# First loads of a one-core kernel: query loads alone on ScalarE's queue, key-value products in three parts, dummy products in TensorE's first waits

## What is computed

```
kv  = einsum('bhsd,bhse->bhde', k, v)             # 8 batches, 8 heads, 576 rows, 64 wide
out = einsum('bhsd,bhde->bhse', q, kv)
x   = out / sqrt(mean(out*out, -1) + 1e-6) * g_norm     # heads side by side: 4608 x 512
x   = relu(x @ w_in)**2 @ w_out                   # 512 -> 2048 -> 512
logits = x @ w_gate + modality_bias[modality_id]; e = argmax(logits)
out[token] = softmax(logits)[e] * (relu(x @ w1[e]) @ w2[e])   # 8 experts, 512 -> 1024 -> 512
```

## Time and profile before

| | us |
|---|---|
| median of 3 runs | 1384.91 (1383.55 to 1385.52) |
| time of the profiled execution | 1386.27 |
| its span in the trace | 1384.4 |
| TensorE busy in the span | 1356.5 (98%) |
| TensorE weight loads busy | 1114.6 (81%) |
| VectorE busy | 814.8 (59%) |
| ScalarE busy | 566.7 (41%) |
| GpSimd busy | 496.8 (36%) |
| mean granted TensorE clock | 0.994 of full |

### The profile page before, as it was taken

The page is one execution under the profiler, slowest core; times in us unless marked ns, Lnnn a source line. Parts: engine busy times, 40 slices in busy tenths (PEclk is TensorE's granted clock), DMA queues, the critical chain, the costliest instruction groups (busy, mean ns, idle before and its releaser), DMA issues. The chain is left out here.

```text
span 1384.4 us, 20776 instructions
## 1 busy us (share of the span) xinstructions
PE 1356.5 (98%) x6951; PEld 1114.6 (81%) x6951; DVE 814.8 (59%) x1765; ACT 566.7 (41%) x1129; POOL 496.8 (36%) x589
## 2 busy tenths in 40 slices
PE   5999999999999999999999999998999999999997
PEld 5887888888888888888887887876788888888876
DVE  3456574574564673664564655546666666666665
ACT  3443334334243333333333333334445545455543
POOL 2643232222132132232232134504555555555541
PEclk9999999999999999999999999999999999999999
DMA  8644646657566666567465464778996113851260
GB/s 231 185 107 151 198 116 199 189 128 201 183 126 190 186 142 199 174 133 215 158 145 161 148 143 160 199 263 199 321 345 243 47 49 115 303 206 48 81 253 21
DMA packets 183398, 237.45 MB, mean 172 GB/s; under 512 B 58734, under 2 KB 101646, under 8 KB 183314
## 3 DMA queue, kind: packets, MB, share of 16 engines
q1 hardware_dynamic: 169010, 214.85, 52.4%
q0 software_dynamic: 9472, 19.96, 4.5%
q10 hardware_dynamic: 4832, 1.57, 0.5%
HBM read 148.07 MB, written 89.30 MB: 171 GB/s over the span
## 5 line engine op out<-in xcount | busy, mean ns | idle before, releaser
L670 POOL TENSOR_TENSOR stage<-stage,stage_hi 128x512 f32<-128x512 f32 x128 | 170.5, 1332 | 547.8 <-ACT stage_hi L1150 547.6
L1499 DVE TENSOR_TENSOR g_sb<-g_sb 128x512 f32<-128x512 f32 x144 | 101.3, 703 | 322.7 <-ACT g_hi L1214 322.7
L1212 ACT ACTIVATE g_sb<-ps_h 128x512 f32<-128x512 f32 x144 | 86.1, 598 | 425.5 <-PE ps_h L817 224.8
L815 PE MATMUL ps_y<-g_hi,weights 128*128 128x512 f32 x576 | 231.0, 401 | 0.0
L815 PE MATMUL ps_h<-xT_hi,weights 128*128 128x512 f32 (+1 forms) x580 | 230.6, 398 | 0.0
L817 PE MATMUL ps_h<-xT_hi,weights 128*128 128x512 f32 (+1 forms) x580 | 225.8, 389 | 0.0
L816 PE MATMUL ps_h<-xT_lo,weights 128*128 128x512 f32 (+1 forms) x580 | 225.5, 389 | 0.0
L817 PE MATMUL ps_y<-g_hi,weights 128*128 128x512 f32 x576 | 224.9, 390 | 0.0
L816 PE MATMUL ps_y<-g_lo,weights 128*128 128x512 f32 x576 | 224.6, 390 | 0.0
L1240 ACT ACTIVATE kv_sb<-ps_h 32x256 f32<-32x256 f32 x384 | 143.9, 375 | 123.2 <-PE ps_h L1002 110.7
L1002 PE MATMUL ps_y<-weights,xT_hi 128*128 128x512 f32 x656 | 177.8, 393 | 0.7 <-DVE xT_lo L1680 0.7
(11 more groups left out here) (269 smaller groups left out, 1764.4 us busy)
## 6 DMA issues: line engine op xcount, KB each, us to landing
stage<-in_moe_w SPq DMA_DIRECT2D x128, 256.0 KB, 2.9
w_hi<-stage_hi SPq DMA_DIRECT2D x128, 256.0 KB, 2.5
w_lo<-stage SPq DMA_DIRECT2D x128, 256.0 KB, 2.9
weights<-w_hi SPq DMA_DIRECT2D x32, 1024.0 KB, 7.1
weights<-w_lo SPq DMA_DIRECT2D x32, 1024.0 KB, 7.2
rows<-y_sb SPq DMA_DIRECT2D x36, 256.0 KB, 9.3
q_sb<-in_q SPq DMA_DIRECT2D x28, 256.0 KB, 3.2
k_sb<-in_k SPq DMA_DIRECT2D x28, 160.0 KB, 3.4
```

Source lines behind the costliest of these rows:

```text
L670: pool.tensor_tensor(stage[n % 2][:, :], stage[n % 2][:, :], stage_hi[n % 2][:, :].bitcast(F32), ALU.subtract).then_inc(split_lo, 1)
L815: pe.matmul(out_ap, lhs[0], rhs[0], start=start, stop=False)
L1212: act.activation(g_sb[:, :], ps_h[c % 2][:, 0:GROUP], ACT.Relu).then_inc(h_read, 1)
L1499: dve.tensor_tensor(g_sb[:, :], g_sb[:, :], g_sb[:, :], ALU.mult).then_inc(g_done, 1)
```

## The change

The query loads stay on ACT, and pieces 0 and 1 move to SP, ahead of pieces 2 to 7. ACT gets one small activation on 8 columns of `ones` (its result is not used) behind the query loads. Keys times values go to two banks (pair 2 to `ps_h[1]`, the others to `ps_a`), and DVE copies them in three takes: pairs 0 and 1, pair 2, pair 3. TensorE's stream is reordered: pair 2 comes before query tile 1, pair 3 after the products of pairs 0 and 1 of tiles 0 to 2. 12 products `ones` x `ones` go ahead of everything and 23 between the last head products and the transposes of x.

```
-            for n in range(2, AHEAD):
+            for n in range(AHEAD):
                 load_own_piece(n)
...
-            for hp in range(2):
-                pe.wait_ge(kv_in[hp], 32)
-                multiply_kv(hp, k_first[hp], v_first[hp])
-            pe.wait_ge(made, 5)
-            pe.wait_ge(first_q_in[0], 16)
-            transpose_tile(ps_qT_first[0], q_first[0], qT_ps)
-            for hp in range(2, HP):
-                pe.wait_ge(first_kv_in[hp - 2], 32)
-                multiply_kv(hp, k_first[hp], v_first[hp])
-            for t in range(1, TILES):
+            def keep_busy(n, out_bank):
+                for _ in range(n):
+                    pe.matmul(out_bank[:, 0:P], ones[:, :], ones[:, :], start=True, stop=True)
+            def first_product_kv(hp):
+                pe.wait_ge(kv_in[hp] if hp < 2 else first_kv_in[hp - 2], 32)
+                multiply_kv(hp, k_first[hp], v_first[hp], ps_kv_first[hp])
+            def first_qT(t):
                 pe.wait_ge(first_q_in[t], 16)
                 transpose_tile(ps_qT_first[t], q_first[t], qT_ps)
+            pe.wait_ge(made, 2)
+            keep_busy(FIRST_BUSY, ps_h[1])
+            for hp in range(2):
+                first_product_kv(hp)
+            pe.wait_ge(made, 5)
+            first_qT(0)
+            first_product_kv(2)
+            first_qT(1)
+            first_qT(2)
+            pe.wait_ge(qT_done, 1)
+            first_qT(3)
+            pe.wait_ge(first_taken, 1)
+            for t in range(TILES - 1):
+                pe.wait_ge(qT_done, t + 1)
+                multiply_heads(Group(0), t, qT_first[t], ps_heads_first[t], (0, 1))
+            first_product_kv(3)
+            pe.wait_ge(qT_done, TILES)
+            multiply_heads(Group(0), TILES - 1, qT_first[TILES - 1], ps_heads_first[TILES - 1], (0, 1))
+            pe.wait_ge(first_taken, 2)
+            for t in range(TILES):
+                multiply_heads(Group(0), t, qT_first[t], ps_heads_first[t], (2,))
             pe.wait_ge(kv_done, 1)
             for t in range(TILES):
-                pe.wait_ge(qT_done, t + 1)
-                multiply_heads(Group(0), t, qT_first[t], ps_heads_first[t])
+                multiply_heads(Group(0), t, qT_first[t], ps_heads_first[t], (3,))
+            keep_busy(NORM_BUSY, ps_y[3])
...
-            for n in range(2):
-                fetch_own_piece(act, n)
+            act.wait_ge(made, 2)
+            act.activation(lg[:, 2, 0, :], ones[:, 0:E], ACT.Copy)
...
-            dve.wait_ge(kv_ps, HP)
-            take_kv(Group(0))
+            for hps in FIRST_TAKES:
+                dve.wait_ge(kv_ps, hps[-1] + 1)
+                for part in range(2):
+                    rows = slice(part * DH, (part + 1) * DH)
+                    last = dve.tensor_copy(kv_sb[0][rows, hps[0]:hps[-1] + 1, rows],
+                                           chunks(ps_kv_first[hps[0]][:, :])[rows, hps[0]:hps[-1] + 1, rows])
+                last.then_inc(kv_done if hps[-1] == HP - 1 else first_taken, 1)
```

More of the change, by code:

```diff
@@ L257, in routed_mlp_program @@
         ps_qT_first, ps_heads_first, ps_xT_first = (
-            (ps_h[0], ps_h[1], ps_y[3], ps_y[2]), (ps_b, ps_y[0], ps_y[1], ps_h[0]), (ps_y[3], ps_y[2], ps_a, ps_h[1]))
+            (ps_h[0], ps_y[3], ps_y[2], ps_h[0]), (ps_b, ps_y[0], ps_y[1], ps_h[0]), (ps_y[3], ps_y[2], ps_a, ps_h[1]))
+        FIRST_TAKES = ((0, 1), (2,), (3,))
+        ps_kv_first = (ps_a, ps_a, ps_h[1], ps_a)
         ps_qT, ps_heads, ps_xT = (ps_a, ps_a, ps_b, ps_a), (ps_b, ps_a, ps_b, ps_a), (ps_b, ps_a, ps_b, ps_a)
@@ L344, in routed_mlp_program @@
         spread_ps, tables_made = sem("spread_ps"), sem("tables_made")
+        first_taken = sem("first_taken")
         passed = sem("passed")
@@ L413, in routed_mlp_program @@
         MADE = 14
+        FIRST_BUSY, NORM_BUSY = 12, 23
         NORM_STEPS = 13
@@ L850, in kv, with multiply_kv @@
                 pe.wait_ge(kv_in[hp % 2], a.count(HP * 32, (hp // 2 + 1) * 64 - FIRST_KV))
-                multiply_kv(hp, k_sb[hp % 2], v_sb[hp % 2])
-            def multiply_kv(hp, k_from, v_from):
+                multiply_kv(hp, k_sb[hp % 2], v_sb[hp % 2], ps_a)
+            def multiply_kv(hp, k_from, v_from, out_bank):
                 steps = k_from.shape[2]
@@ L857, in multiply_kv @@
                         rows = slice(head * DH, (head + 1) * DH)
-                        last = pe.matmul(ps_a[rows, hp * P + head * DH:hp * P + (head + 1) * DH], k_from[:, head, j, :],
+                        last = pe.matmul(out_bank[rows, hp * P + head * DH:hp * P + (head + 1) * DH], k_from[:, head, j, :],
                                          v_from[:, head, j, :], start=(j == 0), stop=(j == steps - 1))
@@ L880, in heads, with multiply_heads @@
                 multiply_heads(a, t, tile_T[:, :, :], ps_heads[t])
-            def multiply_heads(a, t, qT_from, out_bank):
-                for hp in range(HP):
+            def multiply_heads(a, t, qT_from, out_bank, hps=range(HP)):
+                for hp in hps:
                     for batch, lo, hi in q_parts(a, t):
@@ L886, in multiply_heads @@
                                          start=True, stop=True)
-                last.then_inc(heads_ps, 1)
+                if HP - 1 in hps:
+                    last.then_inc(heads_ps, 1)
             def transpose_x(a, t):
```

## The result

| | before | with the change |
|---|---|---|
| median of 10 runs, us | 1384.89 (1383.44 to 1385.60) | 1388.70 (1386.76 to 1390.69) |
| profiled execution, us | 1386.27 | 1388.41 |
| its span, us | 1384.4 | 1386.7 |
| start of the first 512-wide product, us | 35.87 | 39.99 |

The ratio is 1.0026, with a 95% interval of 1.0017 to 1.0035: the changed kernel is slower by 3.6 to 3.8 us. The forecast was +1.7 with "within 0.2%" as the likeliest; the result falls just outside, on the slower side, which had a chance of 0.14, and the measured median lies 0.2 above the top of the range. The first 512-wide product starts 4.12 us later, more than the whole loss.

A forecast was written before the change was run, and what follows sets the result against it. Loads bound the opening until 18.63 us, then TensorE's clock and DVE. Terms +1.8, +1.15 and -1.25 sum to +1.7 us: 1384.91 becomes 1386.6 us, with 8 in 10 for 1383.3 to 1388.5.

The forecast's parts named there:

- the yardstick: Start of the first 512-wide product, 35.87 us before; the opening's gain or loss should reach the end one to one.
- the landing of query tile 3: Last query tile's load, just before 18.63 us; moving pieces 0 and 1 to SP shifts it by 0 (-1.9 to +0.5).
- The clock of the opening: TensorE's clock before the heads: any gain from the opening dummies lost before 18.63 us, rise to 2.4 GHz at 22.4.
- the middle of the two ends: Clock rise taken as 22.4 us, between 20.6 (about as before) and 24.2 (5.6 after work resumes at 18.63).
- The rule that each slow microsecond costs half a one: From 18.63 us, heads end at 23.56 with a fast clock; each microsecond at the slow clock adds half a microsecond.
- The term, +1.8: End of the heads at 25.45 instead of 23.65 us, with pair 3 on the path and the clock rising at 22.4.
- The heads finishing together: Between heads' end and first transpose of x: small steps start 2.55 us after the end instead of 1.39, +1.15.
- The later dummies: 46 records before the transposes of x keep 2.4 GHz: first transpose to 512-wide product 6.15 us instead of 7.41, -1.25.
- The cover behind them: The later dummy records end at 30.45 us, 0.95 ahead of the first transpose of x at 31.4; direct cost 0.
- the held clock: Rival: the clock stays fast from the opening dummies on, heads end at 23.56, sum -0.2, total 1384.7 us; chance 0.18.
- Early queries: Rival: query tiles land early, heads could start 2.7 us earlier, sum -1.0, total 1383.9 us; chance 0.12.
- The slower side: Rival: clock rises later than 24.6 us, total passes +2.8; at 26.0 it is +3.5, 1388.4 us; chance 0.11.

The follow-up runs named there:

- its three variants: The changed kernel with pieces 0 and 1 back on ScalarE (ratio 1.0022), without opening dummies (1.0015), or with pair 3 ahead of query tile 3 (1.0014).
- the filled kernel: The kernel before, its order and queues kept, with dummy products in every wait (12, 9, 3, 6, 6 and 20); ratio 0.9996.

## Why the prediction was right in three terms and short by a fourth

*Moving the yardstick to the 512-wide product was right.* On average over two traces each it moved by 3.8 us, as the medians did.

*The step that failed* is the landing of query tile 3. I took 0 for it, with ends of -1.9 and +0.5, since packets went out one for one and SyncE's queue ahead of it was unchanged. It was +2.2. I looked for the cause in the two queues, and the runs found it in the other edit: the opening dummies, to which I gave a direct cost of "0, at most 0.1" because their records end before pair 0 lands. They did end before (5.74 against 7.10), yet the tile lands 1.5 us later with them in five of six traces. An instruction load of 16 KB, which the dummies bring forward into the last packets of the queries, goes with it in each of the five. In the changed kernel it accounts for about 1.1 us of the shift (all but the last packets have started by 18.6, the last starts at 19.65). The rest is smaller: the other packets started up to 0.7 us later than in the kernel before (17.9), as they did in some traces without dummies (18.6). A rival for a load delayed by the dummies was missing, and no term for instruction loads.

*The clock of the opening.* That it would be lost again before the heads was right, and the trace shows it (0.50 from 11.5 to 20.8). The rise was expected 3.8 us after the tile's start, and came 3.9 us after it, at 24.8 instead of 22.4 since the tile was late. That the middle of the two ends was hit is partly luck: in the other traces with the changed order it ranged from 2.7 to 4.9 us. The rule that each slow microsecond costs half a one gives 4.93 + 3.9 / 2 = 6.9 us for the stretch, measured 7.07: the rule was 0.2 short, and 0.14 to 0.25 in the other traces that kept the order. The term, +1.8 against +2.05, was 0.25 short. By the Trainium skill's page "TensorE: Matmul & The Clock Gate", in its sections on the clock gate, activity releases the slow clock and a long wait between bursts brings it back. The runs agree with the first part: pair 0 took 0.92 us behind the dummies and 1.55 without them. On the second they differ, and the measurement decides: the clock fell at 11.1 us behind waits of only 1.36 and 2.74 us, on either side of pair 0's small products, well short of the 4.8 us of waiting that I had used as a measure.

*The heads finishing together*: +1.15 forecast, +1.11 measured, and +1.10 alone.

*The later dummies*: -1.25 forecast, -1.27 measured, -1.27 and -1.26 alone. The cover behind them was 0.78 us, 0.95 forecast.

*Of the rivals*, the held clock would have given -0.2. In the filled kernel the clock was held by dummies in every wait, 36 ahead of the heads; with the 12 at the start alone it fell in all five traces. Numbers in between were not tried. Early queries did not occur in any trace. The slower side came true in size (+3.6 to 3.8), but not by its mechanism: the rise at 24.8 is just past the mark of 24.6 because the tile was late, not because the clock took longer.

The signs of the four terms say what the change would need to win: it keeps only its last one if the heads stay in tile order, pair 3 stays ahead of query tile 3 and the opening dummies go, and that is the version with the later dummies alone. Its opening is 1.0 to 2.0 us shorter than before in two traces, and its time was not told apart from that of the kernel before (ratios 0.9988 and 1.0004).

## What to carry to other kernels

When TensorE waits on the last of a row of loads, dummy products in earlier waits can only pay if the clock lasts until that load arrives; here it fell in the gaps between small products long before, and the load itself came later. Look at the instruction queue too when an edit adds instructions to an opening that waits for loads: one instruction load of 1.2 us can hold up the last packets of a transfer. Dummies in the last long wait before dense work, sized by the wait's own row, are the ones that shortened the opening here, by 1.3 us in its rows; a gain in the total was not shown. And regrouping products so that several results finish at once moves their whole evacuation behind the last product: count it as one stage, not as something already overlapped.

## What was not expected of the hardware

- With 24 records of `ones` x `ones` on TensorE between 1.45 and 6.7 us, a query load of 256 KB issued at 4.4 us took 15.9 to 16.2 us in five of six traces, against 14.2 to 15.0 in eight traces without them. In those five a 16 KB packet on the instruction queue, 1.2 us long, starts at 16.1 to 18.3 us, before the queries are through, and the last query packets come when it is done; in the others it starts at 18.4 or later and holds up none. Whose instructions these are isn't shown, and data, shape and place of the dummies were not varied by themselves.
- The clock's rise is not tied to the work alone. After query tile 3's transposes began it took 3.9 and 2.7 us in the two traces of the changed kernel, and 2.7, 4.8 and 4.9 us in its three variants; half of such a difference, 0.6 us between the two traces of the changed kernel, goes into the opening with nothing changed.
